# Value windows loaded as 128 rows with zeros, and block means placed behind the loads: two batches of attention, experts and mixer on one core

## What is computed

```python
block, window = (32, 16)
k_sum = k.reshape(B, H, nb, block, D).max(axis=3)
v_sum = v.reshape(B, H, nb, block, D).mean(axis=3)
scores_l = scale * np.matmul(q, k.transpose(0, 1, 3, 2))
mask_l = np.abs(pos[:, None] - pos[None, :]) < window
scores_s = scale * np.einsum('bhsd,bhnd->bhsn', q, k_sum)
scores_s = scores_s + np.log(block)
scores_l_m = np.where(mask_l, scores_l, -1000000000.0)
scores_all = np.concatenate([scores_l_m, scores_s], axis=-1)
scores_all = scores_all - np.max(scores_all, axis=-1, keepdims=True)
a = np.exp(scores_all)
a = a / (np.sum(a, axis=-1, keepdims=True) + 1e-09)
v_all = np.concatenate([v, v_sum], axis=2)
return np.matmul(a, v_all).astype(np.float32)
```

## Time and profile before

| | |
|---|---|
| median of 3 executions | 451.85 us (450.61 to 452.22) |
| the profiled execution | 452.24 us, span in the profile 450.4 us |
| busy: TensorE / VectorE / ScalarE / GpSimd | 431.9 / 298.1 / 227.6 / 134.7 us |
| HBM read | 31.99 MB |
| VW loads | 12 of 384 KB, median 9.6 us from issue to landing |
| SyncE issues VW loads 1 to 4 of the first batch at | 4.01, 5.88, 7.10 and 18.16 us |
| SyncE issues VT 2 at, the first transfer of means at | 16.09, 15.06 us |

### The profile page before, as it was taken

One profiled execution on the slowest core, in us unless ns is written; L12 is line 12 of the kernel. 1 busy time (PEld: TensorE's weight loads), 2 busy tenths in 40 slices (PEclk: granted clock), 3 DMA queues, 4 the chain that ended last, 5 costly groups with the idle time before them and its releaser, 6 DMA issues.

```text
span 450.4 us, 8603 instructions
## 1 busy us (share of the span) xinstructions
PE 431.9 (96%) x3332; PEld 367.1 (81%) x3332; DVE 298.1 (66%) x549; ACT 227.6 (51%) x591; POOL 134.7 (30%) x170
## 2 busy tenths in 40 slices
PE   8799998998997999999999999999999999999997
PEld 3478996887765789978876899998998898989885
DVE  4794489866467835697666877576675776475453
ACT  6785647766237955677782562434443233233120
POOL 3878583000006412000259056631132022200000
PEclk9989998999999999999999999999999999999999
DMA  8965065000493140000022111122123063201103
GB/s 255 261 190 162 26 179 207 1 2 0 123 287 102 25 142 1 0 1 1 1 95 95 47 48 46 49 93 57 46 87 93 0 235 93 72 24 48 47 2 140
DMA packets 13914, 38.12 MB, mean 85 GB/s; under 512 B 1536, under 2 KB 2480, under 8 KB 13872
## 3 DMA queue, kind: packets, MB, share of 16 engines
q1 hardware_dynamic: 13008, 35.98, 26.2%
q10 hardware_dynamic: 864, 1.57, 0.9%
HBM read 31.99 MB, written 4.72 MB: 81 GB/s over the span
## 4 chain that ended last, share of the span: by engine, by line
PE 85%; DVE 8%; ACT 3%; issue 3%; POOL 0%; ACTq 0%; DVEq 0%; POOLq 0%
PE ps_s L683 34%; PE ps_o L683 19%; PE ps_x L683 14%; PE ps_t L683 10%; PE ps_t L855 4%; PE ps_t L750 2%; ACT PA L1094 2%; DVE nmaxM L1443 1%; DVE nmaxA L1351 1%; PE ps_x L869 1%; DVE QS L1391 0%; DVE PTA L1371 0%; DVE PTM L1454 0%; DVE gate_gt L1423 0%; PE ps_s L936 0%
## 5 line engine op out<-in xcount | busy, mean ns | idle before, releaser
L1331 ACT ACTIVATE HID_h<-HID_raw 128x384 fp32r<-128x384 f32 x48 | 25.1, 525 | 72.3 <-DVE HID_raw L1659 31.3
L632 POOL TENSOR_TENSOR W_raw<-W_raw 128x256 f32<-128x256 f32 x11 | 10.7, 975 | 99.3 <-DMA W_raw<-in_ch 88.6
L1094 ACT ACTIVATE PA<-ps_s,biasA 128x120 f32<-128x120 f32 x96 | 33.7, 381 | 12.7 <-DVE biasA L1355 10.1
L683 PE MATMUL ps_s<-C_h,HID_l 128*128 128x512 f32 x96 | 37.7, 393 | 0.0
L683 PE MATMUL ps_s<-C_l,HID_h 128*128 128x512 f32 x96 | 37.7, 393 | 0.0
L683 PE MATMUL ps_s<-C_h,HID_h 128*128 128x512 f32 x96 | 37.6, 392 | 0.0
L547 POOL TENSOR_TENSOR PA<-PA,denA 128x480 f32<-128x480 f32 x24 | 23.7, 986 | 46.7 <-DVE denA L1364 46.6
L1648 DVE SCALAR_TENSOR_TENSOR HID_l<-HID_raw,HID_h 128x384 fp32r<-128x384 f32 x48 | 28.3, 593 | 10.5 <-ACT HID_h L1331 8.1
L1157 ACT ACTIVATE PM<-ps_s,nmaxM 128x128 f32<-128x128 f32 (+5 forms) x48 | 30.1, 634 | 9.5 <-DVE nmaxM L1443 9.0
L683 PE MATMUL ps_o<-V_h,W_h 128*128 128x384 f32 x96 | 32.8, 342 | 0.1
L683 PE MATMUL ps_o<-V_h,W_l 128*128 128x384 f32 x96 | 32.4, 337 | 0.0
(11 more groups left out here) (255 smaller groups left out, 1269.1 us busy)
## 6 DMA issues: line engine op xcount, KB each, us to landing
W_raw<-in_ch SPq DMA_DIRECT2D x12, 512.0 KB, 3.8
C_raw<-in_ch SPq DMA_DIRECT2D x12, 512.0 KB, 3.8
VW<-in_vw SPq DMA_DIRECT2D x12, 384.0 KB, 9.6
KP<-in_kT SPq DMA_DIRECT2D x8, 384.0 KB, 6.4
VT<-in_vT SPq DMA_DIRECT2D x8, 384.0 KB, 6.4
out_x<-US SPq DMA_DIRECT2D x12, 256.0 KB, 2.0
QT<-in_qT SPq DMA_DIRECT2D x7, 384.0 KB, 7.7
raw<-in_tok SPq DMA_DIRECT2D x4, 384.0 KB, 3.3
```

Source lines behind the costliest of these rows:

```text
L632: pool.tensor_tensor(W[S3], W[A11], W[A21], ALU.subtract).then_inc(w_sum, 1)
L683: return pe.matmul(out, lhsT, rhs, start=start, stop=stop)
L1094: last = act.activation(PA[:, u % NPA, j, :], ps_s[u % 2][:, j % 2, (j // 2) * KC:(j // 2 + 1) * KC], ACT.Exp, bias=biasA[:, u % 4, j:j + ...
L1331: act.activation(*own(s, n, half), ACT.Relu).then_inc(g_hi, 1)
```

## The change

VW gets 128 rows. The host pads the value windows from 96 to 128 rows with zeros, so each of the six loads of a batch writes all 128 partitions and carries 512 KB instead of 384 KB. A load now also writes zeros where the means go. Everything that writes means must therefore come behind the load of that window: ScalarE's `a_means` and GpSimd's `copy_means` wait for it, and `place_means` takes a load's index i, waits for that load, and writes the means of that load's windows alone. The first batch has five such transfers instead of two, the second five instead of two, and there is a semaphore for each, for which TensorE waits at the first unit of each group of windows. Value products read rows 0 to 119 as before. In SyncE's order of the first batch, VT 2 and VT 3 move ahead of the first transfer of means, and the fifth VW load ahead of wq.

```diff
-        VW, p = at("VW", [KC, 2, NW, 4 * D], F32, region4)
+        VW, p = at("VW", [P, 2, NW, 4 * D], F32, region4)
...
-        ld_vs = [sem(f"ld_vs{q}") for q in range(2)]
+        ld_vs = [[sem(f"ld_vs{q}{i}") for i in range(3)] for q in range(2)]
...
-                sp.dma_start(VW[0:WK, q, 4 * i:4 * i + 4, :],
+                sp.dma_start(VW[:, q, 4 * i:4 * i + 4, :],
                              vw_d[b, :, q, 4 * i:4 * i + 4, :]).then_inc(ld_vw[q][i], 16)
...
-            def place_means(b, q):
+            def place_means(b, q, i):
 
                 sp.wait_ge(a_vs, 2 * b + q + 1)
-                n = first_placed(b, q)
-                sp.dma_start(VW[WK:KC, q, n:NW, :],
-                             VS[WK:KC, q, :].unsqueeze(1).broadcast_to([NB, NW - n, 4 * D])).then_inc(ld_vs[q], 16)
+                sp.wait_ge(ld_vw[q][i], b * 16 + 16)
+                n, end = max(first_placed(b, q), 4 * i), 4 * i + 4
+                sp.dma_start(VW[WK:KC, q, n:end, :],
+                             VS[WK:KC, q, :].unsqueeze(1).broadcast_to([NB, end - n, 4 * D])).then_inc(ld_vs[q][i], 16)
...
             load_windows(0, 0, 2)
-            place_means(0, 0)
             for r in range(2, PAIRS):
                 load_values(0, r)
+            place_means(0, 0, 1)
             load_weights(0)
+            place_means(0, 0, 2)
             load_queries(0, 1)
-            load_windows(0, 1, 0)
+            for i in range(2):
+                load_windows(0, 1, i)
             load_weights(1)
-            place_means(0, 1)
-            load_windows(0, 1, 1)
+            place_means(0, 1, 0)
+            load_windows(0, 1, 2)
+            place_means(0, 1, 1)
             load_weights(2)
-            load_windows(0, 1, 2)
+            place_means(0, 1, 2)
...
                 for q in range(2):
-                    place_means(b, q)
+                    for i in range(1 - q, 3):
+                        place_means(b, q, i)
...
                 w = DIRECT[0] + 2 * i
+                pool.wait_ge(ld_vw[0][w // 4], 16)
                 pool.tensor_copy(VW[WK:KC, 0, w:w + 2, :],
...
-                if t == first_placed(b, q) // 2:
-                    pe.wait_ge(ld_vs[q], b * 16 + 16)
+                if t >= first_placed(b, q) // 2 and (t % 2 == 0 or t == first_placed(b, q) // 2):
+                    pe.wait_ge(ld_vs[q][t // 2], b * 16 + 16)
...
-                                  VW[:, q, 2 * t + half, j * D:(j + 1) * D],
+                                  VW[0:KC, q, 2 * t + half, j * D:(j + 1) * D],
...
                 n = first_direct(b, q)
+                act.wait_ge(ld_vw[q][0], b * 16 + 16)
                 act.activation(VW[WK:KC, q, 0:n, :], sums.unsqueeze(1).broadcast_to([NB, n, 2 * P]), ACT.Copy,
...
     vw = vw.reshape(B, WK, NW, 2, 4 * D).transpose(0, 1, 3, 2, 4)
+    vw = np.pad(vw, ((0, 0), (0, P - WK), (0, 0), (0, 0), (0, 0)))
```

## The result

The changed kernel took 449.74 us in the median of 13 executions (449.04 to 451.10), the kernel before 451.34 beside it (13, 449.70 to 452.43). The ratio is 0.9964, with a 95% interval of 0.9951 to 0.9978: 0.4% faster, which the measurement tells apart from no change, but less than the 0.5% that I set as a bound. The profiled execution took 449.9 us (span 448.1); that of before 452.24 (450.4).

A forecast was written before the change was run, and what follows sets the result against it. TensorE, busy 96%, was taken as the bound up to 28.74 us, stalled and half-clocked behind slow loads, then ScalarE and VectorE. Maxima 2.0 us earlier, added steps and second batch nothing: 451.85 gives 449.9 us, range 448.0 to 453.3.

The forecast's parts named there:

- What a load costs: VW loads: 128 rows take 1.30 us against 1.62 for 96 rows, 0.32 us less each; bad end 2.1 us.
- the fourth rival: VW loads: a 128-row load lasts 1.62 us like a 96-row one; time 451.9 to 453.8 us, chance 0.04.
- Third VW load and VT: First batch's loads: third VW load lands at 18.0 to 19.8 us for 20.8, VT 2 at 19.0 to 20.8.
- The stall: TensorE's 2.22 us in value tile 1, read as waiting for instructions: restart about 1 us earlier, idle 1.2 us.
- The half clock at 23 us: TensorE's clock of 0.50 for 23 to 26 us, behind the stall: expected gone, 1.3 us saved.
- Maxima 2.0 us earlier: VectorE's maxima of score tile 6 begin at 21.3 us for 23.35; exponentials then at 22.2 for 24.24.
- Steps added: New waits for VW loads and six more transfers of means: cost nothing; bad end of ScalarE's copy minus 0.5 us.
- a cover of some 3 us: ScalarE's second-half means copy: its load lands at about 24 us, 27.3 at the latest, against a need of 26.8.
- The second batch: Loads from 118 us on: through long before that batch's attention at 140 to 150 us, so worth nothing.
- It passes on whole: Between the halves TensorE is the chain, so the 2.0 us gained before reach the end in full.
- the second rival: A second fall of the clock, at 68 to 79 us, also goes: 1.3 us more, time 448.6 us, chance 0.17.
- The first and third rival: First: stall and half clock stay, 451.6 us, chance 0.22; third: instructions come later behind moved loads, 453.6 us, chance 0.13.

The follow-up runs named there:

- the run with less in front of it: Kernel before with the first batch's third VW load issued behind the means, VT 2 and VT 3; median 451.67 us, ratio 0.9997.
- before again: Kernel before, run once more unaltered for a second profile; median 452.45 us, ratio 0.9989 to the other executions of the same kernel.
- VT ahead: Kernel before with VT 2 and VT 3 issued ahead of the first placing of means, 96-row loads kept; median 452.02 us, ratio 1.0013.
- the whole order put back: Changed kernel, 128 rows kept, with SyncE's issues of the first batch in the order of the kernel before; median 451.03 us, ratio 0.9988.
- the old order of the second half: Changed kernel with only SyncE's issues for the first batch's second half in the order of before; median 450.71 us, ratio 0.9980.
- the sums late: Changed kernel with VectorE's last two value sums one tile later, `SUMS_AT = (6, 7)` for `(5, 6)`; median 450.60 us, ratio 0.9971.
- changed again: Changed kernel, run once more unaltered for a second profile; median 449.94 us, ratio 0.9958 to the kernel before.

## Why the prediction was right

The time was right (449.9 for 449.74), and so was its cause in the large: quicker loads end waits of the first batch's attention, and with 96-row loads in the changed kernel the gain is gone. The closeness is partly luck. The gain is 1.6 us beside 451.34, for 2.0 forecast from a median of 451.85, and the two errors nearly cancel. And the 2.0 us were read from an execution with a gap and two falls of the clock, while about half of the executions of before have no fall at all. Several steps had the wrong size or the wrong standing.

**What a load costs: right for most loads.** 1.30 us was taken from 402 GB/s; the mixed stretches move 379 to 415 GB/s and the last three VW loads of the second batch 420, so 0.524 MB takes 1.25 to 1.38 us. The first three of that batch, at 326 GB/s, take 1.61 us, the 1.62 of the fourth rival; nobody waits for them. In 10 to 15 us, where it counts, it is 410 GB/s for 280 before, and the rival falls. What I made of the Trainium skill's port rule ("SBUF — State Buffer", Door 1: The DMA port swizzle), that a load lasts the same with 96 rows and with 128, thus fails for the full column in most stretches. From 96 to 112 rows, which by the same working last the same too, the trace agrees, with 1.57 and 1.59 us.

**Third VW load and VT: right in direction, earlier than my range.** The piece of means that waits for the third load was issued at 17.54, so the load was through by then (its last part landed at 17.02); I had 18.0 to 19.8. VT 2 landed at 19.37, before VectorE got to it at 21.09, and no wait for it is left.

**The stall: wrong, though it did not show in the sum.** I read 2.22 us as a property of the kernel and expected 1.2 us of it to stay. It is gone, but in the second profile of before it was not there either. That it is TensorE's instruction packet fits what was seen (1.4 to 1.5 us from its end to the matmul, in three executions with a gap and one at its edge), but nothing was changed to test it. That the packet waits for the queue's loads is only likely: it is earlier and less scattered with 128 rows, yet VT 2 and VT 3 ahead of it did not delay it, and the run with less in front of it could not tell.

**The half clock at 23 us: gone as forecast, but not tied to the gap as I had it.** With the third load late it is at 0.50 in 23 to 26 us behind waits for GpSimd of 1.24 and 1.51 us and no gap at the packet; with 96 rows everywhere and in the first half alone there are gaps of 0.85 and 0.57 us, and the clock stays at 1.00 there. In none of the eight profiles with 128 rows in the first half does it fall before 72 us, in three of the six with 96 rows it does (at 22.8, 23.0 and 31.7).

**Maxima 2.0 us earlier: 1.4 by their time, 2.1 by the length.** Expected were exponentials at 22.2; they came at 22.99, with everything 0.85 us late from the start. The lengths of the two profiles differ by 26.05 - 23.98 = 2.07 us, against 2.0. Against the two 96-row profiles without gap or fall (24.83 in before again, 24.49 with VT ahead) it is 0.6 to 0.9 us. All executions without a fall differ by 1.4 us in the median, so these two profiles show less than the typical gain, and the median is a mix.

**Steps added: right only for this order and these rows.** The waits and pieces were costed at nothing "with a cover of some 3 us" on ScalarE's copy. The changed kernel has no such wait. The two pieces of means issued at 15.91 and 17.54 landed at 19.7 and 22.2, in time. But with 96 rows the cover was short by 1.78 us, with the whole order put back by 0.58, and with the old order of the second half a piece came 0.40 us late; that kernel's median is 0.8 us higher, with overlapping intervals. I had not seen that moving the second VW load ahead of the first piece pays for the waits. Neither part of the change is told apart from the kernel before by itself: 128 rows in the old order 0.9988 (up to 1.0007), the order with 96 rows 1.0008, both together 0.9964.

**The second batch: right.** 450.28 for 449.94 with 96 rows there.

**It passes on whole: right, and the rest of the profiles' difference is the second rival.** Of the spans' 2.3 us, 36.69 - 35.47 = 1.2 are there at 35 us. Another 1.0 is the half clock near 74 us: from TensorE's second restart there to the end it takes 376.5 us in the three executions that have it (450.4 - 73.92 in before) and 375.4 to 375.6 in all others but one (448.1 - 72.61 = 375.5 in changed; 376.1 with the sums late). (The restart is the end of TensorE's second gap there.) The second rival thus came true for this pair of profiles, with 1.0 us for the 1.3 that I had. It isn't the change's doing in full: one kernel with 128 rows has it too:

```profile
73.00:75.00 2.00, 2.00 (x12) 1.67 (x12) 1.87 (x5) 0.77 (x3) 0.00 (x0) 0.50 0.00 0
```

**The first and third rival** fall: the stall did not stay, and with VT 2 and VT 3 in front the packet ended at 17.5 in the changed kernel, 1.9 us before VT 2 landed.

## What to carry to other kernels

Look at GB/s beside the DMA share: a full share at 60 or 70% of the rate that other loads of the kernel reach is a form of transfer worth changing, even at the price of moving zeros, wherever someone waits for it. When waits for loads are added on a queue, move the next loads ahead of the first such wait. Take a second profile of the same kernel before a stall of two microseconds goes into a sum.

## What the hardware showed that I had not expected

- A packet of the same size takes longer when loads of 96 or 112 rows are in the queues: in 10 to 15 us those of 4,096 bytes (the VW rows) took 256 ns in the mean before and 163 after, those of 3,072 bytes (rows of keys, queries and VT, loaded as 128 rows in both kernels) 171 and 121. So the loads of 128 rows that run between them are slowed as well. Why a full column of rows makes the difference stays open.
- Executions of one kernel differ by 5.9 us (449.22 to 455.09, 122 executions of before, median 451.8; one more took 456.64), those of changed by 2.1 (449.04 to 451.18, 25 executions): the change narrows the spread. With 128 rows in the first half 17 of 85 executions have a fall of the clock, with 96 rows more than half (82 of 157).
- The granted clock fell to 0.50 near 74 us in 3 of 14 profiled executions and cost 1.0 us each time. It isn't set by the idle time before it alone: changed again has gaps of 1.13 and 0.59 us there and stays at 1.00, before had 1.14 and 0.59 and fell.
- The third score tile starts at 10.7 to 11.8 us with 128 rows and at 10.3 to 11.4 with 96, 0.4 us later in the mean. Whether the larger loads delay the first keys, or it is chance in 14 executions, stays open; it would be a price of the change, and is in its median.
